# Attention and two MLPs on one core: first loads in runs of tokens, products of the identity between TensorE's first jobs, another order of the first jobs and of the weights

## Chip, cores and metric

One core of a Trainium2 chip runs the whole program. The metric is device time in microseconds (us), the median of the runs of one kernel. The profile is of one execution. Its times count from the start of its span. The engines are PE (TensorE), DVE (VectorE), ACT (ScalarE), POOL (GpSimd) and SP (SyncE, which here only issues DMAs).

## What is computed

Inputs are float32: q, k and v are 2 x 8 heads x 768 tokens x 64. Three parts follow one another:

```
scores_l = q k^T / 8, kept where |i - j| < 16, else -1e9
scores_s = q max_over_blocks_of_32(k)^T / 8 + log 32
a = softmax(concat(scores_l, scores_s)); x = a concat(v, mean_over_blocks(v))
x -> (1536 x 512);  h = x @ w_in1;  x = (max(h,0) + alpha min(h,0)) @ w_out1
h = x @ w_in2;  g = (a0 + a1 h + a2 h^2 + a3 h^3) / (1 + |b0||h| + |b1|h^2);  out = g @ w_out2
```

w_in is 512 x 2048 and w_out 2048 x 512 in both MLPs.

## The kernel before, in words

Tokens are taken in four chunks of 384 (two halves of each of the two batches). An attention job is one pair of heads of one chunk: 16 jobs, of which 0 to 3 are chunk 0. A job has the stages KQ (L879: keys and queries are transposed on PE into PSUM, `transposes` at L871, and copied to `kt` and `qt` by ACT, L545; DVE takes the maxima over blocks, L736), KX (L896, the same for the keys that lie past the chunk's window, DVE at L743 and L731), SC (L903: scores, 12 products; DVE adds the mask and finds the maximum, L756; ACT takes the exponential, L571), NM (DVE divides by the sum, L760), TR (L913: the probabilities are transposed, ACT copies them to `pt`, L579), AV (L919: means of the values by one product with `avg`, copied by ACT in SU, L580), and PV (L926: 12 products with the values, ACT writes `x_hi` and DVE `x_lo`, L588 and L772).

The MLPs are computed in split precision: each weight is a high part (ACT, L597 and L603) and a low part (POOL, L505 and L510), and each product of 128 x 384 is three matmuls (L948 to L950). An MLP step i works on one tile f = i mod 16 of the hidden dimension: `hidden1(i)` is 12 matmuls, `output1(i - 2)` another 12. From step 0 on, the stages of the next chunk's jobs lie in slots between them. For chunk 1 `SOON` (L66) puts job 4's KQ in step 0, SC in step 2, TR and PV in step 3. In step f of chunk 0 ACT does the slots' work, then makes the high parts of some weights (`weights`, L664 to L668), and then copies `g1_hi` of the step (L673), all in this order. Before, step 2 makes the weights of tiles 5 and 6, step 3 those of 7 and 8, and step f from 4 on that of f + 5.

Chunk 0's four jobs have nothing to lie beside. Their stages run in three orders written out by hand, one list for each of PE, ACT and DVE (`FIRST_PE`, `FIRST_ACT`, `FIRST_DVE`, L69 to L78), with the products of `hidden1(0)` and `hidden1(1)` (HD) at PE's end, and the high parts of the weights 0 to 2 (WI, WO) in ACT's. Each of the four jobs has PSUM banks of its own. POOL makes the identity, which PE's transposes need, and the constants, then adds up the values of each pair (L472), then splits weights; `keep_first_sums` (L494) follows the first two.

SP issues every DMA in one order (L370 to L423). `load_pair` (L265) makes two DMAs, one for each head. In them each partition gets one token of each tile, so every packet is 64 floats (256 B). `load_w(0, n)` loads the weights of the tiles 2n and 2n + 1 (1 MB). `load_keys(5)` waits until PE has transposed the keys of job 4 (L286), and `load_values(4)` waits for `pool_v0` (L335), which `keep_first_sums` raises.

Of the kernel before, what the change touches and what calls it, by code (L numbers as in the profile page):

```python
# [13 lines left out]
def attention_two_mlps(nc, q, k, v, w_in1, w_out1, alpha, w_in2, w_out2, a_coef, b_coef, out):  # L14
# [10 lines left out]
    B, H, S, D = q.shape  # L25
    DM, DF = w_in1.shape
    P = 128
# [41 lines left out]
    FIRST_PE = [(0, KQ), (0, KX), (1, KQ), (0, SC), (1, KX), (2, KQ), (0, AV), (1, SC), (2, KX), (0, TR), (3, KQ),  # L69
                (2, SC), (1, TR), (1, AV), (0, PV), (3, KX), (2, AV), (3, SC), (2, TR), (3, AV), (1, PV), (2, PV),  # L70
                (3, TR), (0, HD), (3, PV), (0, HD), (0, HD), (0, HD), (1, HD), (1, HD), (1, HD), (1, HD)]

    FIRST_ACT = [(0, KQ), (1, KQ), (0, SC), (2, KQ), (0, SU), (1, SC), (0, TR), (3, KQ), (1, TR), (2, SC), (1, SU), (0, PV),
                 (2, SU), (0, WI), (2, TR), (3, SC), (1, PV), (3, SU), (3, TR), (2, PV), (1, WI), (3, PV),
                 (2, WI), (0, WO), (1, WO), (2, WO)]

    FIRST_DVE = [(0, KQ), (0, KX), (1, KQ), (0, SC), (1, KX), (0, NM), (2, KQ), (1, SC), (2, KX), (1, NM), (2, SC),
                 (3, KQ), (3, KX), (2, NM), (0, PV), (3, SC), (3, NM), (1, PV), (2, PV), (3, PV)]  # L78
# [25 lines left out]
    k_raw0 = place("k_raw0", [P, 4, H, D], offset=w_end - 4 * H * D * 4)  # L104
    kx_raw0 = place("kx_raw0", [P, 4, H, D], offset=w_end - 8 * H * D * 4)
    q_raw0 = place("q_raw0", [P, QTILES, H, D], offset=w_end - (8 + QTILES) * H * D * 4)
# [49 lines left out]
    with ExitStack() as ctx:  # L156
# [107 lines left out]
        def _(sp):  # L264
# [4 lines left out]

            def first_k(p):  # L270
                hs = heads(p)
                load_pair(k_raw0[:, :, hs, :], KROWS[0], k[0, hs, 0:4 * KROWS[0], :], k0_loaded[p])

            def first_q(p):
                hs = heads(p)
                load_pair(q_raw0[:, :, hs, :], P, q[0, hs, 0:CH, :], q0_loaded[p])

            def first_kx(p):
                hs = heads(p)
                load_pair(kx_raw0[:, :, hs, :], KXROWS, k[0, hs, 4 * KROWS[0]:S, :], kx0_loaded[p])  # L280
# [94 lines left out]
            first_rest(0)  # L375
            first_kx(1)
            first_k(2)
            first_q(2)
            first_rest(1)
            first_k(3)  # L380
            first_kx(2)
            first_q(3)
            first_rest(2)
            first_windows(0)
            first_edges()
            first_kx(3)
            first_rest(3)
            load_w_in(0, 0)
# [150 lines left out]
        def _(act):  # L539
# [109 lines left out]
            for i in range(STEPS):  # L649
# [14 lines left out]
                if c == 0:  # L664

                    for n in (f + 3,) if f < 2 else (2 * f + 1, 2 * f + 2) if f < 4 else (f + 5,):
                        if n < FT:
                            weights(0, n)  # L668
# [419 lines left out]
```

## Time and profile before

| | us |
|---|---|
| median of 3 runs | 626.73 |
| lowest and highest | 626.6, 627.32 |
| the profiled execution | 627.17 |
| its span | 625.5 |
| TensorE busy | 608.0 |
| from the start to the end of step 0's products | 39.37 |
| the longest gap of TensorE after that, before 350 us | 3.22 |

A page of the profile has busy times, a line of 40 slices, and the chain of work that ended last. The windows give the same for any stretch, with the clock that was granted to TensorE, as a share of its full 2.4 GHz (0.50 is 1.2 GHz). In the timeline a row is one instruction or several alike: start, duration, engine, line, operation, tile written and tiles read, count, and in brackets how long the engine had been idle and what released it. A product of float32 tiles (L910, L925, L938) shows as two MATMUL rows, a transpose (L875, L917) as one.

### The profile page before, as it was taken

The numbers are of one execution on the slowest core, as the hardware profiler recorded it, in microseconds if no ns is written. First come the engines' busy times: TensorE is split into PE (matmuls) and PEld (weight loads), VectorE is DVE, ScalarE is ACT, GpSimd is POOL, SyncE is SP. The second block draws the span as 40 slices with busy tenths as digits, with TensorE's granted clock in tenths as the row PEclk, the third lists the DMA queues.
The fourth block names the chain that finished last, engine by engine and source line by source line (L and its number), as shares of the span: only waits on it lengthen the run. The fifth ranks groups of instructions, "written<-read, shape, count | busy, mean of one in ns | idle before, by whom it ended". The sixth has DMA issues, their size and how long they took to land.

```text
span 625.5 us, 10573 instructions
## 1 busy us (share of the span) xinstructions
PE 608.0 (97%) x3897; PEld 566.8 (91%) x3897; DVE 415.2 (66%) x953; ACT 312.7 (50%) x778; POOL 196.9 (31%) x221
## 2 busy tenths in 40 slices
PE   6897999999999999999999999999999999999997
PEld 4787999999999999999999989998998999899996
DVE  3663555556655554555555599877987788778775
ACT  4785453243223432332443487557656666656654
POOL 5467548000000000000322376443344334434431
PEclk9898999999999999999999999999999999999999
DMA  8979717202220222001444300001000000001001
GB/s 180 235 193 286 176 27 136 46 18 63 62 50 7 46 50 51 2 1 35 135 135 135 102 1 1 1 0 52 0 2 1 34 18 1 0 2 50 1 2 50
DMA packets 79539, 37.30 MB, mean 60 GB/s; under 512 B 56496, under 2 KB 72896, under 8 KB 79296
## 3 DMA queue, kind: packets, MB, share of 16 engines
q1 hardware_dynamic: 79488, 36.63, 23.1%
q8 instruction: 31, 0.51, 0.3%
q14 instruction: 20, 0.16, 0.1%
HBM read 32.58 MB, written 3.15 MB: 57 GB/s over the span
## 4 chain that ended last, share of the span: by engine, by line
PE 92%; SPq 3%; DMA 1%; DVE 1%; ACT 1%; issue 1%; ACTq 0%
PE acc L948 15%; PE acc L950 14%; PE acc L949 14%; PE hid L948 11%; PE hid L950 10%; PE hid L949 10%; PE att L948 4%; PE att L950 4%; PE att L949 4%; SPq L268 2%; PE att L938 2%; PE att L875 1%; PE att L910 1%; PE att L917 1%; DMA w_out_raw<-in_moe_w_out_dram 1%; DMA kx_raw<-in_k_dram 1%
## 5 line engine op out<-in xcount | busy, mean ns | idle before, releaser
L948 PE MATMUL hid<-x_hi,w_in_hi 128*128 128x384 f32 x384 | 130.7, 340 | 0.0
L950 PE MATMUL hid<-x_hi,w_in_lo 128*128 128x384 f32 x384 | 129.3, 337 | 0.0
L949 PE MATMUL hid<-x_lo,w_in_hi 128*128 128x384 f32 x384 | 129.3, 337 | 0.0
L510 POOL TENSOR_TENSOR w_out_lo<-w_out_raw,w_out_hi 128x512 fp32r<-128x512 f32 x32 | 41.3, 1292 | 226.1 <-ACT w_out_hi L541 225.9
L948 PE MATMUL acc<-g_hi,w_out_hi 128*128 128x384 f32 x256 | 91.0, 356 | 0.0
L531 POOL TENSOR_SCALAR qpart<-habs,ab 128x384 f32<-128x384 f32 x64 | 44.0, 688 | 143.1 <-ACT poly L690 142.4
L950 PE MATMUL acc<-g_hi,w_out_lo 128*128 128x384 f32 x256 | 86.8, 339 | 0.0
L949 PE MATMUL acc<-g_lo,w_out_hi 128*128 128x384 f32 x256 | 86.5, 338 | 0.0
L541 ACT ACTIVATE g_hi<-hid 128x384 fp32r<-128x384 f32 x96 | 48.3, 503 | 69.3 <-PE acc L950 62.0
L788 DVE TENSOR_TENSOR g_lo<-hid,g_hi 128x384 fp32r<-128x384 f32 x64 | 35.6, 556 | 69.3 <-ACT g_hi L541 69.3
L950 PE MATMUL acc<-w_out_hi,g_lo 128*128 128x512 f32 x192 | 76.1, 396 | 0.0
L949 PE MATMUL acc<-w_out_lo,g_hi 128*128 128x512 f32 x192 | 75.6, 394 | 0.0
L948 PE MATMUL acc<-w_out_hi,g_hi 128*128 128x512 f32 x192 | 75.5, 393 | 0.0
L948 PEld LDWEIGHTS hid<-x_hi,w_in_hi 128*128 128x128 f32 x384 | 72.3, 188 | 1.9 <-DVE x_lo L772 0.4
L949 PEld LDWEIGHTS hid<-x_lo,w_in_hi 128*128 128x128 f32 x384 | 72.4, 189 | 1.3
L950 PEld LDWEIGHTS hid<-x_hi,w_in_lo 128*128 128x128 f32 x384 | 72.3, 188 | 0.0
L811 DVE TENSOR_SCALAR g_neg<-hid,prelu_alpha 128x384 f32<-128x384 f32 x64 | 39.4, 615 | 46.0 <-PE hid L950 46.0
L533 POOL TENSOR_TENSOR qpart<-qpart,habs 128x384 f32<-128x384 f32 x64 | 65.7, 1026 | 5.3
L948 PEld LDWEIGHTS acc<-g_hi,w_out_hi 128*128 128x128 f32 x256 | 48.0, 188 | 2.7 <-issue 1.7
L949 PEld LDWEIGHTS acc<-g_lo,w_out_hi 128*128 128x128 f32 x256 | 48.2, 188 | 0.0
L950 PEld LDWEIGHTS acc<-g_hi,w_out_lo 128*128 128x128 f32 x256 | 48.1, 188 | 0.0
L571 ACT ACTIVATE att<-att,nmax 128x120 f32<-128x120 f32 x78 | 24.7, 367 | 45.8 <-DVE nmax L756 45.8
(155 smaller groups left out, 1150.5 us busy)
## 6 DMA issues: line engine op xcount, KB each, us to landing
w_in_raw<-in_moe_w_in_dram SPq DMA_DIRECT2D x32, 256.0 KB, 4.3
w_out_raw<-in_moe_w_out_dram SPq DMA_DIRECT2D x16, 512.0 KB, 4.5
vw<-in_v_dram SPq DMA_DIRECT2D x32, 120.0 KB, 3.9
q_raw<-in_q_dram SPq DMA_DIRECT2D x32, 96.0 KB, 2.6
out_dram<-out_sb SPq DMA_DIRECT2D x12, 256.0 KB, 2.0
k_raw<-in_k_dram SPq DMA_DIRECT2D x16, 104.0 KB
k_raw<-in_k_dram SPq DMA_DIRECT2D x16, 100.0 KB
vs_raw<-in_v_dram SPq DMA_DIRECT2D x2, 768.0 KB, 7.9
```

Of the source, the lines that this page charges most:

```text
L268: sp.dma_start(dst[0:rows, :, h, :], src[h].rearrange("(t p) d -> p t d", p=rows)).then_inc(loaded, 16)
L510: pool.tensor_tensor(w_out_lo[:, f, :], w_out_raw[:, f, :], w_out_hi[f][:, :].bitcast(F32), ALU.subtract).then_inc(pool_w_out, 1)
L531: pool.tensor_scalar(qpart[:, i % 2, :], habs[:, i % 2, :], ab[:, 5:6], ab[:, 4:5], ALU.mult, ALU.add).then_inc(pool_qb, 1)
L533: pool.tensor_tensor(qpart[:, i % 2, :], qpart[:, i % 2, :], habs[:, i % 2, :], ALU.mult).then_inc(pool_q, 1)
L541: return act.activation(dst, src, ACT.Identity)
L571: last = act.activation(scores_of(bk, h, n), scores_of(bk, h, n), ACT.Exp, scale=-1.0, bias=nmax[:, s, i:i + 1], accum_out=sums_of(bk, h)[ ...
L788: dve.tensor_tensor(g1_lo[:, i % R1, :], hid[i % 2][:, 0:CH], g1_hi[:, i % R1, :].bitcast(F32), ALU.subtract).then_inc(dve_g, 1)
L811: dve.tensor_scalar(g_neg[:, :], hb, 0.0, prelu_alpha[:, f:f + 1], ALU.min, ALU.mult).then_inc(dve_m, 1)
L938: last = pe.matmul(bk[0][rows, u * QT:(u + 1) * QT], values, pt[0:KU, s, h * UP + u // 2, tokens], start=True, stop=True)
L948: pe.matmul(dst, lhs[0], rhs[0], start=start, stop=False)
L949: pe.matmul(dst, lhs[0], rhs[1], start=False, stop=False)
L950: return pe.matmul(dst, lhs[1], rhs[0], start=False, stop=stop)
```

## The change

The first loads of keys and queries become one DMA for each pair, in which a partition gets a run of 4 (queries: 3) neighbouring tokens of each head. What a transpose writes then goes to every fourth (third) column. The two heads are transposed one by one, by a product with the identity whose result has 64 partitions. Products of the identity with itself, 15 in all, are issued ahead of four of PE's first jobs, into a bank that is not yet used. The three lists and SP's order are new, and in chunk 0 ACT makes the weights of tile f + 3 in step f, one tile in each step.

```diff
     SOON = {(0, 2): [KQ], (2, 0): [SC], (2, 2): [NM], (3, 0): [TR], (3, 2): [PV]}
-    FIRST_PE = [(0, KQ), (0, KX), (1, KQ), (0, SC), (1, KX), (2, KQ), (0, AV), (1, SC), (2, KX), (0, TR), (3, KQ),
-                (2, SC), (1, TR), (1, AV), (0, PV), (3, KX), (2, AV), (3, SC), (2, TR), (3, AV), (1, PV), (2, PV),
-                (3, TR), (0, HD), (3, PV), (0, HD), (0, HD), (0, HD), (1, HD), (1, HD), (1, HD), (1, HD)]
-    FIRST_ACT = [(0, KQ), (1, KQ), (0, SC), (2, KQ), (0, SU), (1, SC), (0, TR), (3, KQ), (1, TR), (2, SC), (1, SU), (0, PV),
-                 (2, SU), (0, WI), (2, TR), (3, SC), (1, PV), (3, SU), (3, TR), (2, PV), (1, WI), (3, PV),
+    FIRST_PE = [(0, KQ), (0, KX), (1, KQ), (0, SC), (1, KX), (1, SC), (2, KQ), (0, AV), (0, TR), (2, KX), (3, KQ),
+                (1, AV), (2, SC), (1, TR), (3, KX), (2, AV), (0, PV), (3, SC), (2, TR), (1, PV), (3, AV), (3, TR),
+                (2, PV), (3, PV), (0, HD), (0, HD), (0, HD), (0, HD), (1, HD), (1, HD), (1, HD), (1, HD)]
+    RUN_UP = {(0, KQ): 5, (0, KX): 3, (1, SC): 4, (0, AV): 3}
+    FIRST_ACT = [(0, KQ), (1, KQ), (0, SC), (2, KQ), (1, SC), (0, SU), (0, TR), (3, KQ), (1, SU), (1, TR), (2, SC),
+                 (2, SU), (0, PV), (2, TR), (3, SC), (0, WI), (3, SU), (3, TR), (1, PV), (2, PV), (1, WI), (3, PV),
                  (2, WI), (0, WO), (1, WO), (2, WO)]
-    FIRST_DVE = [(0, KQ), (0, KX), (1, KQ), (0, SC), (1, KX), (0, NM), (2, KQ), (1, SC), (2, KX), (1, NM), (2, SC),
-                 (3, KQ), (3, KX), (2, NM), (0, PV), (3, SC), (3, NM), (1, PV), (2, PV), (3, PV)]
+    FIRST_DVE = [(0, KQ), (0, KX), (1, KQ), (1, KX), (0, SC), (1, SC), (0, NM), (2, KQ), (1, NM), (2, KX), (3, KQ),
+                 (2, SC), (3, KX), (2, NM), (3, SC), (0, PV), (3, NM), (1, PV), (2, PV), (3, PV)]
     top = (nc.sbuf_base + 31) // 32 * 32
...
     w_in_raw = place("w_in_raw", [P, FT, KD, P], offset=top)
     w_in_lo = place("w_in_lo", [P, FT, KD, P], F32R)
     w_end = top + FT * DM * 4
-    k_raw0 = place("k_raw0", [P, 4, H, D], offset=w_end - 4 * H * D * 4)
-    kx_raw0 = place("kx_raw0", [P, 4, H, D], offset=w_end - 8 * H * D * 4)
-    q_raw0 = place("q_raw0", [P, QTILES, H, D], offset=w_end - (8 + QTILES) * H * D * 4)
+    k_raw0 = place("k_raw0", [P, H, 4, D], offset=w_end - 4 * H * D * 4)
+    kx_raw0 = place("kx_raw0", [P, H, 4, D], offset=w_end - 8 * H * D * 4)
+    q_raw0 = place("q_raw0", [P, H, QTILES, D], offset=w_end - (8 + QTILES) * H * D * 4)
     w_out_hi = [place(f"w_out_hi{f}", [P, DM], F32R) for f in range(FT)]
     w_out_raw = place("w_out_raw", [P, FT, DM], offset=top)
     w_out_lo = place("w_out_lo", [P, FT, DM], F32R)
...
                 for h in range(2):
                     sp.dma_start(dst[0:rows, :, h, :], src[h].rearrange("(t p) d -> p t d", p=rows)).then_inc(loaded, 16)
+            def load_runs(dst, rows, src, loaded):
+                sp.dma_start(dst[0:rows, :, :, :].rearrange("p h t d -> p h (t d)"),
+                             src.rearrange("h (p t) d -> p h (t d)", p=rows)).then_inc(loaded, 16)
             def first_k(p):
                 hs = heads(p)
-                load_pair(k_raw0[:, :, hs, :], KROWS[0], k[0, hs, 0:4 * KROWS[0], :], k0_loaded[p])
+                load_runs(k_raw0[:, hs, :, :], KROWS[0], k[0, hs, 0:4 * KROWS[0], :], k0_loaded[p])
             def first_q(p):
                 hs = heads(p)
-                load_pair(q_raw0[:, :, hs, :], P, q[0, hs, 0:CH, :], q0_loaded[p])
+                load_runs(q_raw0[:, hs, :, :], P, q[0, hs, 0:CH, :], q0_loaded[p])
             def first_kx(p):
                 hs = heads(p)
-                load_pair(kx_raw0[:, :, hs, :], KXROWS, k[0, hs, 4 * KROWS[0]:S, :], kx0_loaded[p])
+                load_runs(kx_raw0[:, hs, :, :], KXROWS, k[0, hs, 4 * KROWS[0]:S, :], kx0_loaded[p])
             def load_keys(j):
                 b, hs, n = batch(j), heads(pair(j)), KROWS[half(j)]
...
             first_kx(0)
             first_k(1)
             first_q(1)
-            first_rest(0)
             first_kx(1)
             first_k(2)
+            first_rest(0)
+            first_kx(2)
             first_q(2)
             first_rest(1)
             first_k(3)
-            first_kx(2)
             first_q(3)
             first_rest(2)
+            first_kx(3)
             first_windows(0)
             first_edges()
-            first_kx(3)
             first_rest(3)
-            load_w_in(0, 0)
             first_windows(1)
             sp.dma_start(alpha_rows[0:FT, :], alpha.rearrange("(f p) -> f p", p=P)).then_inc(alpha_loaded, 16)
+            load_w_in(0, 0)
             first_windows(2)
             first_windows(3)
             load_w_out(0, 0)
...
             load_keys(4)
             load_w_out(0, 1)
             load_w(0, 2)
+            load_w(0, 3)
+            load_values(4)
+            load_w(0, 4)
             load_keys(5)
-            load_values(4)
-            load_w(0, 3)
-            load_w(0, 4)
             load_w(0, 5)
             load_values(5)
             load_w(0, 6)
...
                 slot(c + 1, f, 2)
                 if c == 0:
-                    for n in (f + 3,) if f < 2 else (2 * f + 1, 2 * f + 2) if f < 4 else (f + 5,):
-                        if n < FT:
-                            weights(0, n)
+                    if f + 3 < FT:
+                        weights(0, f + 3)
                 if i >= LAST + LW:
                     weights(1, i - LAST - LW)
                 if i >= R1:
...
                 def transposes(dst, raw, raw0, rows, tiles):
+                    columns = dst[:, 0:rows * tiles].rearrange("p (r t) -> p r t", t=tiles)
                     for t in range(tiles):
-                        rows_of_pair = raw0[0:rows, t, heads(p), :] if first else raw[0:rows, t, :, :]
-                        tr = pe.transpose(dst[:, t * rows:(t + 1) * rows], rows_of_pair.rearrange("p h d -> p (h d)"), ident[0:rows, 0:rows])
+                        if first:
+                            for h in range(2):
+                                tr = pe.matmul(columns[h * D:(h + 1) * D, :, t], raw0[0:rows, 2 * p + h, t, :], ident[0:rows, 0:rows],
+                                               start=True, stop=True)
+                        else:
+                            tr = pe.transpose(dst[:, t * rows:(t + 1) * rows], raw[0:rows, t, :, :].rearrange("p h d -> p (h d)"),
+                                              ident[0:rows, 0:rows])
                     return tr
                 before = j - 1 if j > NPAIR else 0
...
                     if j == 0:
                         pe.wait_ge(pool_ready, 1)
                     if first:
-                        pe.wait_ge(k0_loaded[p], 32)
+                        pe.wait_ge(k0_loaded[p], 16)
                     else:
                         pe.wait_ge(dve_x, before + 1)
                         pe.wait_ge(k_loaded, 32 * (j - NPAIR + 1))
                     transposes(bk[0], k_raw, k_raw0, n, 4).then_inc(pe_k, 1)
                     if first:
-                        pe.wait_ge(q0_loaded[p], 32)
+                        pe.wait_ge(q0_loaded[p], 16)
                         if j == 3:
                             pe.wait_ge(act_su, 1)
                     else:
...
                 elif stage == KX and half(j) == 0:
                     pe.wait_ge(dve_kmax, kx_jobs(j))
                     if first:
-                        pe.wait_ge(kx0_loaded[p], 32)
+                        pe.wait_ge(kx0_loaded[p], 16)
                     else:
                         pe.wait_ge(kx_loaded, 32 * (kx_jobs(j) - NPAIR))
                     transposes(bk[0], kx_raw, kx_raw0, KXROWS, 4).then_inc(pe_kx, 1)
...
                         mm.then_inc(pe_y, 1)
             begun = [0, 0]
+            pe.wait_ge(pool_ready, 1)
             for j, stage in FIRST_PE:
+                for _ in range(RUN_UP.get((j, stage), 0)):
+                    pe.matmul(acc[2][:, 0:P], ident[:, :], ident[:, :], start=True, stop=True)
                 if stage == HD:
                     hidden1(j, [begun[j]])
                     begun[j] += 1
```

## Rows read from the trace of the kernel before

**Rows 1.** The page: busy tenths and granted clock in 40 slices.
```profile
PE   6897999999999999999999999999999999999997
...
PEclk9898999999999999999999999999999999999999
```
**Rows 2.** Windows: stretch, length, busy us of each engine, PEclk, DMA share, GB/s.
```profile
0.00:17.00 17.00, 9.96 (x80) 7.62 (x81) 7.57 (x36) 7.64 (x25) 9.65 (x26) 1.00 0.82 183
...
39.37:50.72 11.35, 11.35 (x87) 10.27 (x86) 6.49 (x24) 7.30 (x24) 8.80 (x8) 1.00 0.67 173
50.72:53.94 3.22, 0.00 (x1) 0.04 (x1) 0.88 (x2) 1.77 (x4) 2.12 (x2) 0.98 1.05 344
53.94:57.40 3.46, 3.46 (x30) 3.34 (x31) 1.33 (x3) 1.88 (x4) 0.79 (x1) 0.52 1.13 330
57.40:67.40 10.00, 10.00 (x80) 9.55 (x80) 5.31 (x20) 4.81 (x16) 6.75 (x6) 1.00 0.99 230
```
**Rows 3.** The chain that ended last: start, us, what.
```profile
46.91 5.09 DMA w_out_raw<-in_moe_w_out_dram
...
73.54 0.85 PE att L938 x24
```
**Rows 4.** Timeline, ACT and PE around 52 us.
```profile
52.02 0.63 ACT L541 ACTIVATE w_out_hi<-w_out_raw 128x512 fp32r<-128x512 f32 x1 [1.75 <-DMA w_out_raw<-in_moe_w_out_dram]
...
52.93 0.86 ACT L541 ACTIVATE pt<-att 120x384 f32<-120x384 f32 x2
...
53.94 1.55 PE L938 MATMUL att<-pt,vw 120*64 120x64 f32 x24 [3.22 <-ACT pt L541]
```
**Rows 5.** Waits of SP's own queue, 0 to 80 us: total, times, longest.
```profile
SPq L268 <- PE att L875: 9.5, 2, 5.1
```
**Rows 6.** Timeline, DVE: first reduction of KX, then all its waits to 36.3 us.
```profile
7.29 0.53 DVE L743 TENSOR_REDUCE att<-att 128x11 f32<-128x352 f32 x1 [0.94 <-PE att L875]
...
9.04 0.60 DVE L736 TENSOR_REDUCE hid<-hid 128x13 f32<-128x416 f32 x1 [0.78 <-ACT kt L541]
...
11.40 0.29 DVE L756 CUSTOM_DVE_ANT_0 att<-att,mask 128x120 f32<-128x120 f32 x1 [1.76 <-PE att L910]
...
17.69 0.53 DVE L743 TENSOR_REDUCE acc<-acc 128x11 f32<-128x352 f32 x1 [0.28 <-PE acc L875]
...
21.74 0.29 DVE L756 CUSTOM_DVE_ANT_0 acc<-acc,mask 128x120 f32<-128x120 f32 x1 [1.40 <-PE acc L910]
...
24.75 0.53 DVE L743 TENSOR_REDUCE acc<-acc 128x11 f32<-128x352 f32 x1 [1.00 <-PE acc L875]
...
28.69 0.29 DVE L756 CUSTOM_DVE_ANT_0 acc<-acc,mask 128x120 f32<-128x120 f32 x1 [0.82 <-PE acc L910]
...
31.55 0.16 DVE L764 TENSOR_SCALAR pden<-acc 128x3 f32<-128x3 f32 x1 [1.31 <-ACT acc L571]
...
35.01 0.56 DVE L772 TENSOR_TENSOR x_lo<-acc,x_hi 128x384 fp32r<-128x384 f32 x1 [1.11 <-ACT x_hi L541]
...
36.21 0.56 DVE L772 TENSOR_TENSOR x_lo<-acc,x_hi 128x384 fp32r<-128x384 f32 x1 [0.65 <-ACT x_hi L541]
```
**Rows 7.** Timeline, start: SP's first loads, identity, TensorE's jobs; scores late.
```profile
0.82 0.87 SPq L268 DMA_DIRECT2D k_raw<-in_k_dram  x2
...
1.25 0.29 POOL L432 TENSOR_SCALAR_AFFINE_SELECT ident<-ident 128x128 f32<-128x128 f32 x1 [0.23 <-POOL ident L430]
...
4.05 0.93 PE L875 MATMUL att<-ident,k_raw 104*128 104x104 f32 x4 [4.05 <-DMA k_raw<-in_k_dram]
...
9.73 1.48 PE L910 MATMUL att<-kt,qt 64*64 64x120 f32 x24
...
21.61 1.53 PE L917 MATMUL hid<-ident,probs 128*120 128x128 f32 x6
...
22.93 0.48 PE L925 MATMUL att<-v_all_early,avg 96*120 96x128 f32 x2
...
64.50 0.85 PE L910 MATMUL att<-kt,qt 64*64 64x120 f32 x24
```
**Rows 8.** Windows of 0.25 us: where the granted clock fell and rose.
```profile
26.50:26.75 0.25, 0.25 (x1) 0.25 (x2) 0.22 (x3) 0.25 (x1) 0.17 (x2) 0.55 1.03 194
...
29.75:30.00 0.25, 0.25 (x3) 0.25 (x2) 0.25 (x4) 0.23 (x1) 0.25 (x1) 0.62 0.89 344
```
**Rows 9.** Windows of 2 us: the DMAs' GB/s (last column).
```profile
2.00:4.00 2.00, 0.00 (x0) 0.00 (x0) 0.00 (x0) 0.10 (x1) 1.71 (x6) 1.00 0.89 201
...
36.00:38.00 2.00, 2.00 (x13) 1.75 (x12) 0.91 (x3) 1.85 (x5) 1.78 (x3) 1.00 0.97 309
```

## The prediction, made before the changed kernel was run

> **What bounds the kernel now.** I read the page first: TensorE is at nine tenths in nearly every slice [rows 1], and from 57.4 us on it has work without a gap until the second MLP. A change that touches the start can only bring that point forward; what follows it keeps its length. So I read the windows up to there [rows 2]. In the first 17 us TensorE is busy for 9.96. Then two losses stand out: from 50.72 to 53.94 it does nothing for 3.22 us, and for the next 3.46 us it works at a granted clock of 0.52 (1.2 GHz for nearly all of it). The page shows the second as the dip in its fourth slice.
>
> The chain and the timeline tell what ended that gap. TensorE waited for ACT's copy of job 4's probabilities, ACT makes that copy only after the high part of weight tile 6, and that one waited for its load, 5.09 us on the chain [rows 3, 4]. The load stood in SP's queue behind the keys of job 5, for which SP waited up to 5.1 us on TensorE's transposes [rows 5]. So it is an order's fault, not bandwidth's.
>
> Before 39.37 us no one engine bounds. DVE comes nearest: from its first reduction of KX at 7.29 to the end of its last x_lo (36.21 + 0.56 = 36.77) it waits nine times, 9.11 us in all [rows 6], so 20.4 us are its own work. TensorE itself runs there at half speed: 12 products of the scores take 1.48 us at 9.73 and 0.85 at 64.50 [rows 7]. The column of the granted clock reads 1.00 at 9.73 all the same; its first recorded change is the fall at 26.5, with the rise at 29.9 [rows 8]. I go by the durations.
>
> **The change part by part.** Durations are of one execution of 627.17 us (span 625.5); the median is 0.44 below it, and I subtract the gain from the median.
>
> *The gap at 50.72.* Tile 6 is now made in step 3, behind TR and PV, and its load goes ahead of load_values(4) and load_keys(5). Both remove the wait. In step 2 ACT then has one tile (two copies) after job 4's exponentials, and the copies of job 4 are out before output1(1) ends at 50.7. TensorE goes straight from output1(1) into PV. That gives back 3.22 us. Since it doesn't stand still, its clock doesn't fall: 3.46 us at 0.52 would be 1.8 at full clock, 1.66 less [rows 2]; by the pieces (PV 1.55 against 0.85 [rows 3, 4], six later products) I get 1.5. I take 1.6, together **4.8**. Bounds: 3.2 if the clock falls anyway, 4.9 at most.
>
> What is late next: load_keys(5), now behind load_values(4) and 1 MB more of weights. At the 230 to 344 GB/s of these stretches [rows 2] that megabyte takes 3 to 4.5 us, and the keys are wanted only in step 4, about 14 us after step 0. SP's wait on TensorE is over by then, so this queue gets shorter. What stands behind a wait for pool_v0 in load_values(4) (load_w(0, 4), load_keys(5)) has the same 14 us. The later tiles are made three steps (some 15 us) ahead of use, and POOL's splitting of tile 4's outgoing weights stands behind tile 6's incoming ones for one step; output1(4) is two steps off. I cost these at nothing.
>
> *The first loads.* Twelve DMAs instead of 24, each issued in 0.43 (two in 0.87 [rows 7]), take 5.2 us off SP's queue, and 1 KB packets replace 256 B ones. The DMAs moved 201 GB/s while only the small packets ran and 309 with the weights' larger ones [rows 9]. I put the new packets near 309; lower bound 201. Keys of job 0 land at about 3.6, not 4.05. A job's three loads are 589 KB, 2.9 us at the one rate and 1.9 at the other, so the fourth job's land about 4 us earlier. At the lower bound the first jobs' end moves by only 0.2 us, because DVE and TensorE then set the pace.
>
> *The transposes of the first four jobs.* Seven for KQ become 14 products and four for KX eight. The trace has no such product. Nearest is PV: 12 products, K 120, 64 outputs, heads on alternate halves of the array, 768 columns in 0.85 us, or 1.55 at the half clock [rows 3, 4]: 1.1 or 2.0 ns a column. Keys (832 columns) then cost 0.92 or 1.6, queries (768) 0.85 or 1.5, KX (704) 0.78 or 1.4, where the old four transposes of keys took 0.93 at the half clock [rows 7]. So at full clock a new one costs what an old one costs at half; at half clock it is dear. Bounds: 0.85 ns, if long columns hide the overhead, and for the strided write in PSUM, which no row shows, up to double.
>
> *The 15 identity products.* The float32 product of AV, 128 columns, takes 0.48 [rows 7]; counted from start to start 0.43 cold, half of it warm. The first five run from 1.6 us, once the identity is there (1.25 + 0.29), to 3.8: 0.2 past the keys' landing. Of the other ten, three delay KX(0) by 0.25 and the rest fill waits. Their cost on the path is 0.4. What they are worth is the clock. It rose at 29.9 after 3.4 us without a gap in AV, SC and TR, and at 57.2 after PV and MLP products [rows 8, 2]; it did not rise between 9.7 and 13.4 us, where TensorE was as full, but mostly with transposes. Now it is full from 1.6 to 8 us, and with products alone. I take the rise at about 6 us; bounds 4 and 12.
>
> The Trainium skill ("TensorE: Matmul & The Clock Gate", PE-mode transpose) says that transposes don't count as activity for this clock. This trace agrees with it for the stretch of 9.7 to 13.4; without the rule a rise as late as 12 us would be as good a guess as 6, and step 0 would end 2.6 later.
>
> *The first jobs worked forward.* Each job gets its duration from these rows and starts at the latest of its engine's previous job and what it waits for, plus 0.07. With the old lists and landings this ends step 0 at 38.75, where the trace has 39.37, so I add 0.6. With the new lists: KQ(0) 3.8 to 6.5, KX(0) 7.2 to 8.0, KQ(1) to 9.8, SC(0) to 10.5, KX(1) to 11.3, SC(1) 12.6 to 13.4, SC(2) ending at 21.4, SC(3) at 25.0. DVE begins KX(0)'s reduction at 8.25, 0.96 later than before. After it come the same 20.4 us of work and waits of 0.74 (keys 1), 1.15 (KX 1), 0.09, 0.67 (SC 2), 0.15, 1.73 (PV 1, behind TR 3) and 0.4, in all 4.9 where there were 9.1. It ends at 8.25 + 20.4 + 4.9 = 33.6, against 36.77. Step 0 ends at 36.4, with the 0.6 at 37.0: **2.4 us earlier**. Of this most is order and landings: with the new lists and loads but the old transposes and clock I get the same 36.5. A warm clock and dearer products nearly cancel.
>
> *Sum:* 2.4 + 4.8 = 7.2 on 627.17; less 0.1 for a hop or two in the slots is 7.1. From the median, 626.73 - 7.1 = **619.6**.
>
> **Rivals.**
>
> *The clock falls once more or rises late* (0.22). Between 24 and 30 us TensorE still has only some 2.5 us of work, with a gap of 1.7. Before, the clock fell at 26.5 after a stretch like it [rows 8]. A fall at 30 makes PV and HD slow and costs 1.3 by the same working; a first rise at 12 instead of 6 costs 2.6. Gain 4.5 to 5.8: 621 to 622.3. Against it: nothing in the list guards that place, so it is quite possible.
>
> *Another wait takes the gap's place* (0.1). ACT in step 3 or PV for its values, whose DMAs now run beside 2 MB of weights: 344 GB/s and a DMA share over 1 in the gap say that the DMAs are full there [rows 2]. A third to a half of the 4.8 would stay: 621.5 to 622.5. If the whole gap stayed and only the first jobs gained, 624.3.
>
> *The new transposes are dearer than PV's products* (0.12), the one on the other side. Each writes every fourth or third column of PSUM. At 1.5 times the price the forward working ends step 0 at 39.4 + 0.6, at double at 43.6 + 0.6, at triple at 52.8 + 0.6. Double makes the change worth 4.8 - 4.8 = 0 (626.7); triple gives 636. It decides from about 1.9 times. Against it: the two heads write different halves, as in PV, and at 1.1 ns a column they write PSUM less often than the MLPs' products do (most of 80 matmuls with 384 columns each in 10 us [rows 2]).
>
> The Trainium skill ("PSUM — Partial Sum Buffer", Specifications) says that any non-contiguous access pattern slows matmuls significantly. No row before shows such a pattern written by TensorE; by that sentence the sum would be this rival's, and its 0.12 is my doubt of it here.
>
> *The change does less than it says* (0.04): the loads in runs land no earlier and the lists wait elsewhere. Only the 4.8 remains: 622.
>
> **How the numbers follow.** The forecast has 0.52; its own bounds (rise at 4 or 8 us, 0.85 ns a column, the middle's 4.5 to 4.9) give 618.3 to 620.8. The range goes down to 617.8 and up to 624.3, over the first two rivals and the milder half of the third. Left out are the whole doubled price and a gain beyond every bound, under 0.2. A measurement can tell 0.2%, 1.25 us, from no change. Slower by more than that needs over twice the price per column: 0.06. Within it: 0.04. Faster: 0.90.
>
> **What would show it.** Right: no wait of TensorE's PV for ACT in step 3, and no DMA wait of ACT at L541 there; a granted clock of 1.00 from 45 to 60; scores of job 0 in about 0.8 us, not 1.48; end of step 0's products at 37 (36 to 39). KX's eight products in 0.7 to 0.9 us warm prove the price; 1.4 or more warm would be the PSUM rival. DVE's waits up to the last x_lo should sum to about 5. A second window of 0.50 near 30 would be the first rival. The forecast is wrong if step 0 ends after 39.4 or any gap over 1 us stands between it and 57 us; from 60 us on both traces should be alike, only shifted.

## The result and the profile after

The changed kernel takes 620.94 us (620.12 to 621.24 in 4 runs), the kernel before 626.79. The ratio is 0.9896, with a 95% interval of 0.9874 to 0.9918. That is 5.85 us less, where 7.1 were forecast (619.6). The profiled execution took 620.91, its span 619.2.

The page of the changed kernel, busy tenths and granted clock:

```profile
PE   8899999999999999999999999999999999999997
...
PEclk9989999999999999999999999999999999999999
```

Before, the clock dips in the second and in the fourth slice [rows 1]. Both dips are gone; one is there in the third slice, at 31 us. Two instructions mark off the stretches in both traces: the first transposes of job 4 (the end of step 0's products) and of job 5 (step 4). First the timeline of PE before, then after:

```profile
39.54 0.51 PE L875 MATMUL att<-ident,k_raw 100*128 100x100 f32 x4
...
58.45 0.51 PE L875 MATMUL att<-ident,k_raw 100*128 100x100 f32 x4
```

```profile
38.06 0.51 PE L886 MATMUL att<-ident,k_raw 100*128 100x100 f32 x4
...
52.22 0.51 PE L886 MATMUL att<-ident,k_raw 100*128 100x100 f32 x4
```

Call the first instant X, the second Y. X comes 1.48 us earlier, the stretch from X to Y shrinks from 18.91 to 14.16, 4.75 less, and from Y to the end of the span it is 567.05 against 566.98. So nothing happened after Y, and 1.48 + 4.75 = 6.23 is the spans' difference to 0.07. The forecast had 2.4 and 4.8.

Windows of the changed kernel (stretch, length, busy us of PE, PEld, DVE, ACT and POOL, PEclk, DMA share, GB/s) answer to those of [rows 2] and to the first 2 us window of [rows 9]:

```profile
0.00:17.00 17.00, 15.11 (x199) 13.10 (x199) 7.07 (x38) 7.01 (x27) 9.31 (x25) 1.00 0.85 209
2.00:4.00 2.00, 2.00 (x10) 1.80 (x9) 0.00 (x0) 0.10 (x1) 1.71 (x6) 1.00 0.75 230
8.00:10.00 2.00, 2.00 (x45) 1.96 (x44) 0.93 (x3) 0.38 (x2) 0.00 (x0) 1.00 1.09 254
31.25:34.50 3.25, 3.25 (x36) 3.00 (x31) 1.66 (x4) 2.61 (x6) 1.76 (x2) 0.50 0.94 222
38.06:52.22 14.16, 14.16 (x122) 13.08 (x121) 8.80 (x29) 9.62 (x29) 8.58 (x7) 1.00 0.98 258
```

From X to Y TensorE is busy without a gap at full clock: the stand at 50.72 and the slow 3.46 us behind it are both gone. From 31.25 on it runs at 1.2 GHz for some 3.3 us. The DMAs in the first stretch move 230 and 254 GB/s, not the 309 that I put them near.

The timeline of DVE after, with its first reduction of KX and the waits until its last x_lo, answers to [rows 6]:

```profile
8.90 0.53 DVE L749 TENSOR_REDUCE att<-att 128x11 f32<-128x352 f32 x1 [1.71 <-PE att L883]
...
10.35 0.60 DVE L742 TENSOR_REDUCE hid<-hid 128x13 f32<-128x416 f32 x1 [0.48 <-ACT kt L548]
...
11.88 0.53 DVE L749 TENSOR_REDUCE hid<-hid 128x11 f32<-128x352 f32 x1 [0.93 <-PE hid L883]
...
20.77 0.60 DVE L742 TENSOR_REDUCE acc<-acc 128x13 f32<-128x416 f32 x1 [0.32 <-ACT kt L548]
...
21.53 0.29 DVE L762 CUSTOM_DVE_ANT_0 acc<-acc,mask 128x120 f32<-128x120 f32 x1 [0.17 <-PE acc L922]
...
28.07 0.16 DVE L770 TENSOR_SCALAR pden<-acc 128x3 f32<-128x3 f32 x1 [0.48 <-ACT acc L578]
...
31.66 0.56 DVE L778 TENSOR_TENSOR x_lo<-hid,x_hi 128x384 fp32r<-128x384 f32 x1 [1.72 <-ACT x_hi L548]
...
33.68 0.56 DVE L778 TENSOR_TENSOR x_lo<-acc,x_hi 128x384 fp32r<-128x384 f32 x1 [1.00 <-ACT x_hi L548]
...
36.25 0.62 DVE L817 TENSOR_SCALAR g_neg<-hid,prelu_alpha 128x384 f32<-128x384 f32 x1 [1.93 <-PE hid L962]
```

The waits up to 34.24 sum to 0.48 + 0.93 + 0.32 + 0.17 + 0.48 + 1.72 + 1.00 = 5.1 (forecast 4.9, before 9.1). They begin from 8.90 (forecast 8.25) and the last x_lo ends at 34.24 (33.6). The last row shows what the slow clock does: DVE stands another 1.93 us for the first hidden tile, whose matmuls run at half speed.

TensorE's early jobs on the timeline after, to set beside [rows 7]:

```profile
4.17 1.66 PE L883 MATMUL att<-ident,k_raw 104*64 104x104 f32 x16
...
8.03 0.83 PE L883 MATMUL att<-ident,kx_raw 88*64 88x88 f32 x16
8.69 0.89 PE L883 MATMUL hid<-ident,k_raw 104*64 104x104 f32 x16
...
10.16 0.84 PE L922 MATMUL att<-kt,qt 64*64 64x120 f32 x24
```

Job 0's scores take 0.84 us instead of 1.48, so the clock is at full speed there; KQ of job 0 still ran slow. A KX of 704 columns takes 0.66 from start to start (8.03 to 8.69), which is 0.94 ns a column.

### The profile page after: what moved, and what is told of

Same layout as the page of the kernel before. It is cut to its first block, busy times and chain, and to the rows that moved or that the text cites. A ratio compares the mean times of both kernels' runs of the same rounds, so it can differ in the third digit from the quotient of the medians.

```text
span 619.2 us, 10885 instructions
## 1 busy us (share of the span) xinstructions
PE 610.2 (99%) x4059; PEld 569.6 (92%) x4059; DVE 414.0 (67%) x953; ACT 311.4 (50%) x778; POOL 197.3 (32%) x221
## 4 chain that ended last, share of the span: by engine, by line
PE 96%; DVE 3%; ACT 0%; issue 0%; POOL 0%; POOLq 0%
PE acc L960 15%; PE acc L962 14%; PE acc L961 14%; PE hid L960 11%; PE hid L962 11%; PE hid L961 11%; PE att L960 4%; PE att L962 4%; PE att L961 4%; PE att L950 2%; PE att L922 2%; PE att L886 2%; PE att L929 1%; PE att L883 1%; PE acc L1047 1%; DVE probs L774 1%
```

## The experiments

Twelve kernels were run, in three groups of four, each group with its own runs of the kernel before: medians of 627.03, 626.81 and 627.10 us there. The kernel before is not very steady on those chips (624.3 to 629.4 in 36 runs); differences under 1 us between kernels of different groups are not read. The first group ran on one chip, the second and the third on another. Each kernel's profile gives X, Y and the span:

| | median | X | Y | Y - X | span - Y | granted clock under 1 before Y |
|---|---|---|---|---|---|---|
| before | 626.79 | 39.54 | 58.45 | 18.91 | 567.05 | 26.5 to 30, 54 to 57 |
| after | 620.94 | 38.06 | 52.22 | 14.16 | 566.98 | 31 to 35 |
| e1: before, weights' order and lead | 621.58 | 38.03 | 52.63 | 14.60 | 566.97 | none |
| e2: after, old order and lead | 626.63 | 37.59 | 58.20 | 20.61 | 566.90 | 30 to 34, 51 to 58 |
| e3: after, no identity products | 621.93 | 39.25 | 53.43 | 14.18 | 566.97 | 29.6 to 36.4 |
| e4: after, six more ahead of TR 3 | 620.78 | 36.42 | 51.27 | 14.85 | 567.03 | none |
| e5: e4, WO 2 in step 0 | 620.25 | 36.00 | 51.55 | 15.55 | 567.15 | none |
| e6: after, neighbouring columns | 621.13 | 36.57 | 51.12 | 14.55 | 567.28 | none |
| e7: after, old lists | 621.22 | 37.61 | 51.77 | 14.16 | 567.13 | 26 to 30 |
| e8: after, old first loads, transposes | 622.42 | 39.03 | 53.20 | 14.17 | 567.00 | 16 to 20, 30 to 37 |
| e9: before, SP's order alone | 621.43 | 38.00 | 53.70 | 15.70 | 567.00 | none |
| e10: before, ACT's lead alone | 621.82 | 37.85 | 53.01 | 15.16 | 566.99 | none |
| e11: e5, keys 5 ahead of weights | 619.26 | 35.74 | 50.42 | 14.68 | 566.98 | none |
| e12: after, again | 620.85 | 38.29 | 52.45 | 14.16 | 566.95 | 31 to 35 |

The column span - Y is the same to 0.4 us in all of them: everything these edits do, they do before Y.

**e1, the weights alone.** The kernel before with

```diff
             load_w(0, 2)
-            load_keys(5)
-            load_values(4)
             load_w(0, 3)
+            load_values(4)
             load_w(0, 4)
+            load_keys(5)
...
-                    for n in (f + 3,) if f < 2 else (2 * f + 1, 2 * f + 2) if f < 4 else (f + 5,):
-                        if n < FT:
-                            weights(0, n)
+                    if f + 3 < FT:
+                        weights(0, f + 3)
```

> The kernel before with only SP's order of the weights and ACT's lead of three tiles changed; the first jobs are untouched. Theory A (the order of the weights is worth what the two traces show between the transposes of job 4 and those of job 5, 18.9 against 14.2 us): 626.8 - 4.7 = 622.1, no gap of PE near 51 us, step 0 ends at 39.4 as before. Rival (the wait comes back elsewhere once the first jobs end late, as loads are late too): over 624.

621.58 us (621.05 to 622.39, 4 runs), ratio 0.9925, interval 0.9902 to 0.9948: 5.45 us less than before. The gap is gone and Y - X is 14.60. X is 38.03 though the first jobs are the old ones, 1.5 earlier than in the profile of before, and no fall of the clock is recorded at 26.5. e9 and e10 (below), which keep the first jobs as well, have X at 38.00 and 37.85, again with no fall. In e10 nothing differs from the kernel before until step 2. In e9 DVE gets job 2's scores at 21.81, where the kernel before has 21.74 [rows 6]; behind the fall they part, and the wait of DVE that ends at 31.55 before ends at 30.03. So 1.5 us of X in the old kernel hang on whether the clock falls there in that execution. The two profiles that the first section compares differ in that as well as in the change.

**e2, the first jobs alone.** The changed kernel with e1's diff undone.

> The changed kernel with the old order of the weights behind load_w(0, 2) and the old lead of ACT. Theory A: only the first jobs' 1.5 us stay, 625.3, and a gap of about 3 us before job 4's PV is back, with the clock's fall behind it. Rival (the loads' lead from the faster start is enough to hide the wait): under 623.

626.63 us (625.24 to 628.95, 10 runs), ratio 1.0003, interval 0.9984 to 1.0021. Theory A held for the gap and missed the time. X is 1.95 us earlier than before, but Y is 58.20, only 0.25 earlier. The timeline of ACT shows why:

```profile
48.92 0.63 ACT L548 ACTIVATE w_in_hi<-w_in_raw 128x512 fp32r<-128x512 f32 x1 [2.78 <-DMA w_in_raw<-in_moe_w_in_dram]
...
51.20 0.63 ACT L548 ACTIVATE w_out_hi<-w_out_raw 128x512 fp32r<-128x512 f32 x1 [1.65 <-DMA w_out_raw<-in_moe_w_out_dram]
...
52.10 0.86 ACT L548 ACTIVATE pt<-att 120x384 f32<-120x384 f32 x2
```

ACT waits 2.78 and 1.65 us for the loads of tile 6, and job 4's copy comes at 52.10, where it came at 52.93 before. So PE stands for 4.34 us ahead of PV instead of 3.22, and the slow clock behind it lasts to 57.7. What ends the gap is a landing, not work. SP asks for job 5's keys 1.95 us earlier (38.13 against 40.08), but its DMAs of job 4's values then take longer to issue, and the load of tile 6's outgoing weights goes out at 46.20 against 46.91. A faster start mostly makes the wait longer. The half of the change that concerns the first jobs is worth nothing measurable without the other half.

**e9 and e10, the two parts of e1.** e9 has SP's order alone, e10 ACT's lead alone.

> The kernel before with SP's new order behind load_w(0, 2) alone; ACT keeps its old lead. Theory A (either half removes most of the gap: the load of tile 6 lands some 6 us earlier, so ACT doesn't wait for it in step 2): 622 to 623. Rival (ACT's two tiles in step 2 are themselves too much work ahead of g1_high(2) and job 4's copies): 624 to 625.5, with a shorter gap at 50 us.

> The kernel before with ACT's lead of three tiles alone; SP keeps its old order. Theory A (tile 6 is asked for in step 3, behind TR, and its load has landed by 52): the gap of PV is gone, but g1_high(3) waits for the load; 622.5 to 624.5. Rival (the wait only moves behind PV and costs the same): 625 to 627.

621.43 us (620.5 to 622.39) and 621.82 (621.67 to 625.32), ratios 0.9902 (0.9879 to 0.9925) and 0.9926 (0.9900 to 0.9953). Both are better than either theory had it, and neither can be told from e1. One of the two is enough. In e10 the load is still late, but it is asked for after the copies. The timeline of ACT in e10:

```profile
47.61 0.87 ACT L541 ACTIVATE pt<-att 120x384 f32<-120x384 f32 x2
...
52.70 0.63 ACT L541 ACTIVATE w_out_hi<-w_out_raw 128x512 fp32r<-128x512 f32 x1 [0.78 <-DMA w_out_raw<-in_moe_w_out_dram]
```

The copies of job 4 come at 47.61, and the wait for tile 6's load has shrunk to 0.78, at a place where PE has hidden1(4) to do. Both profiles have a stand of PE ahead of hidden1(2), behind a late load_w_out(0, 1) for which ACT waits (1.78 us in e9, 1.91 in e10). PE in e9, then in e10:

```profile
40.43 0.41 PE L948 MATMUL hid<-x_hi,w_in_hi 128*128 128x384 f32 x1 [1.59 <-DVE g_lo L788]
```

```profile
39.70 0.41 PE L947 MATMUL hid<-x_hi,w_in_hi 128*128 128x384 f32 x1 [1.01 <-DVE g_lo L787]
```

Without this stand Y - X would be 14.11 in e9 and 14.15 in e10; e1, whose stand is 0.46, has 14.14. That is the 14.16 of the changed kernel, where PE doesn't stand. So each of the two parts takes away the whole gap, and what their profiles have above 14.2 is the landing of load_w_out(0, 1), a limit that e4 meets again.

**e3, no identity products.** The changed kernel with

```diff
-    RUN_UP = {(0, KQ): 5, (0, KX): 3, (1, SC): 4, (0, AV): 3}
+    RUN_UP = {}
```

> The changed kernel without the 15 products of the identity. Theory A (the products bring the clock up at 7 us; without them the new transposes, being products, bring it up some us later): 0.5 to 2 us slower than the changed kernel, 621.5 to 623. Rival B (without them the clock stays at half until 20 us or more, and they are the whole gain of the start): 624 to 626. Rival C (they only fill waits): 620.9.

621.93 us (621.33 to 622.63, 4 runs), ratio 0.9930, interval 0.9907 to 0.9953: about 1 us above the changed kernel's two medians, inside theory A's range, though the intervals touch. The timeline of PE:

```profile
7.21 1.44 PE L883 MATMUL att<-ident,kx_raw 88*64 88x88 f32 x16
8.44 1.20 PE L883 MATMUL hid<-ident,k_raw 104*64 104x104 f32 x16
9.47 0.82 PE L883 MATMUL hid<-ident,q_raw 128*64 128x128 f32 x12
...
28.86 0.54 PE L929 MATMUL acc<-ident,probs 128*120 128x128 f32 x3 [1.21 <-DVE probs L774]
29.80 0.90 PE L929 MATMUL acc<-ident,probs 128*120 128x128 f32 x3 [0.39 <-DVE probs L774]
```

KX takes 1.44 us, then the keys of job 1 1.20 and its queries 0.82: the clock rises during these keys, about 9 us, where with the identity products KX at 8.03 was already fast. That is one to two us later and costs almost nothing, since no identity products stand ahead of KX: scores of job 0 begin at 10.22 against 10.16. The keys of job 0 start at 4.13 here, released by their DMA, and at 4.17 in the changed kernel, just behind the five identity products. The real loss is later. TR of job 3 takes 0.54 for its first half and 0.90 for its second; the clock has fallen at 29.6, and it is back only at 36.4, where the changed kernel is slow from 31.2 to 34.6. X is 1.2 later. Why the fall is longer without the identity products, 20 us behind the last of them, no run shows.

**e4, TensorE kept busy ahead of the fall.** Five more identity products ahead of TR of job 3, one between its halves, into `att[0]`, which is free there:

```diff
                     for g in range(2):
+                        if j == 3 and g == 1:
+                            pe.matmul(att[0][:, 0:P], ident[:, :], ident[:, :], start=True, stop=True)
                         pe.wait_ge(dve_p, 2 * j + g + 1)
...
+                if (j, stage) == (3, TR):
+                    pe.wait_ge(dve_x, 1)
+                    for _ in range(5):
+                        pe.matmul(att[0][:, 0:P], ident[:, :], ident[:, :], start=True, stop=True)
```

> The changed kernel with six more products of the identity: five before job 3's TR and one between its halves, where PE stands for 1.26 and 0.39 us ahead of the clock's fall at 31.2. Theory A (that stand brings the clock down, and the fall costs 1.3 to 1.7 us): the clock stays at full, 619.4. Rival (it falls anyway, since TR counts for little, or the products delay TR): 620.9 or a little above.

620.78 us (620.01 to 621.28, 4 runs), ratio 0.9910, interval 0.9887 to 0.9933. The clock never falls in the profile and X is 36.42, 1.64 us earlier than after: theory A's price of the fall at X, 1.3 to 1.7, is right. The products do hold the clock: e4, e5 and e11, which have them, ran 15 times, and 14 of these have a mean granted clock of 0.999 or 1.000; of the ten runs of the changed kernel without them (e12 among these) two have. But the stand does not bring the clock down each time, since e6 has the same stand, 1.27 and 0.39 us, and no fall in its profile. And the time hardly moves, where theory A had 619.4. Two rows of e4 tell where the gain went, ACT and then PE:

```profile
36.25 0.63 ACT L548 ACTIVATE w_out_hi<-w_out_raw 128x512 fp32r<-128x512 f32 x1 [1.73 <-DMA w_out_raw<-in_moe_w_out_dram]
...
38.00 0.41 PE L962 MATMUL hid<-x_hi,w_in_hi 128*128 128x384 f32 x1 [0.74 <-DVE g_lo L794]
```

ACT now waits 1.73 us for load_w_out(0, 1), the last weight in its first list, so g1 of step 0 is late and PE stands for 0.74 behind job 4's transposes. Y - X is 14.85 instead of 14.16. That takes back 0.7 in this execution; the other three ran 0.5 to 1.3 us longer than the profiled one.

**e5, that weight made later.** e4, and

```diff
-                 (2, WI), (0, WO), (1, WO), (2, WO)]
+                 (2, WI), (0, WO), (1, WO)]
...
+                    if f == 0:
+                        w_out_high(0, 2)
                     if f + 3 < FT:
```

> The kernel of e4 with the high part of outgoing weight tile 2 made in step 0, behind g1_high(0), instead of last in ACT's first list. Theory D (the landing of load_w_out(0, 1) at 36.2 now ends the first stretch: ACT waits 1.7 us for it, g1 of step 0 is late, and PE stands 0.74 us behind job 4's transposes): that stand is gone, 620.0. Rival (the stand moves to output1(0) or job 4's PV, which wait for other loads): 620.8.

620.25 us (619.47 to 621.85, 6 runs), ratio 0.9900, interval 0.9881 to 0.9919. The stand at 38 is gone, and two others are there. The rival was right that it would move, though it named other places. The last of them, on PE:

```profile
51.55 0.53 PE L888 MATMUL att<-ident,k_raw 100*128 100x100 f32 x4 [0.74 <-DMA k_raw<-in_k_dram]
```

PE stands 0.74 us for the keys of job 5, whose load the change put behind load_values(4) and 2 MB of weights, `load_w(0, 3)` and `load_w(0, 4)`. I had cost that order at nothing; with X two us earlier it isn't.

**e11, those keys ahead of the weights.** e5, and

```diff
             load_w(0, 3)
             load_values(4)
-            load_w(0, 4)
             load_keys(5)
+            load_w(0, 4)
```

> The kernel of e5 with load_keys(5) ahead of load_w(0, 4). Theory D (with the first jobs ended at 36, the landings set the next 15 us, and in e5 the last stand of PE, 0.74 us ahead of job 5's transposes, is for these keys): that stand is gone, the distance between the transposes of job 4 and of job 5 falls from 15.6 to 14.6 or less, 619.2. Rival (the DMAs are full and another load is late in its place): 620.2.

619.26 us (618.48 to 619.75, 5 runs), ratio 0.9872, interval 0.9854 to 0.9889. Y is 50.42, the earliest of all. Theory D's time was right; its "14.6 or less" for Y - X is 14.68. Of the stands behind X a wait of ACT for load_w_out(0, 2) and one of PE remain, ACT first:

```profile
39.98 0.63 ACT L548 ACTIVATE w_out_hi<-w_out_raw 128x512 fp32r<-128x512 f32 x1 [0.16 <-DMA w_out_raw<-in_moe_w_out_dram]
...
44.76 0.55 PE L933 MATMUL att<-ident,probs 128*120 128x128 f32 x3 [0.40 <-DVE probs L776]
```

**e12, the changed kernel beside it.**

> The changed kernel itself, unchanged, on the same chip as e9 to e11, so that one round of runs holds it beside them: 620.9, and if theory D holds 1 to 1.7 us above e11.

620.85 us (619.59 to 621.42, 6 runs), ratio 0.9895, interval 0.9878 to 0.9912. e11 is 1.6 us faster by the medians of one chip, the distance that theory D gave. Its slowest run is 0.16 above the fastest of e12, so the two distributions hardly overlap. e11 beats both kernels, by the six products, the later weight and the keys' order together.

**e6, the strided write.** The changed kernel with

```diff
-                    columns = dst[:, 0:rows * tiles].rearrange("p (r t) -> p r t", t=tiles)
+                    columns = dst[:, 0:rows * tiles].rearrange("p (t r) -> p r t", t=tiles)
```

> The changed kernel, in which the new transposes write neighbouring columns, so that the tokens of the first four jobs are in another order than they should be (the first chunk's attention is of other pairs of tokens). Theory A (the strided write costs nothing, the products' 0.85 to 0.94 ns a column is their own price): 88-column products of KX take 0.66 us from start to start as in the changed kernel, time 620.9. Rival (part of the price is the stride): 0.35 to 0.5 us for KX, and up to 1 us faster.

621.13 us (620.15 to 623.11, 4 runs), ratio 0.9914, interval 0.9890 to 0.9938, no gain. The timeline of PE:

```profile
7.98 0.83 PE L883 MATMUL att<-ident,kx_raw 88*64 88x88 f32 x16
8.64 0.89 PE L883 MATMUL hid<-ident,k_raw 104*64 104x104 f32 x16
9.36 0.83 PE L883 MATMUL hid<-ident,q_raw 128*64 128x128 f32 x12
```

KX takes 0.66 us from start to start, as with the stride, and the durations are the same, 0.83, 0.89 and 0.83. Writing every third or fourth column of PSUM costs these products nothing. X was 36.57 here, with no fall of the clock recorded, although PE stands ahead of job 3's TR as in the changed kernel.

**e7, the old lists.** The changed kernel with the three old lists.

> The changed kernel with the three old lists, the identity products kept ahead of the same four jobs. Theory A (the lists matter little once loads and clock are as they are): 620.5 to 621.5. Rival (the lists are what saves DVE's waits): 622 to 623.5.

621.22 us (620.46 to 623.17, 4 runs), ratio 0.9916, interval 0.9892 to 0.9941. Theory A: the new lists alone can't be told from the old. X is 37.61 with a fall of the clock in it, as the new lists have 38.06 with one.

**e8, the old first loads and transposes.** `load_pair` with its 256 B packets, and seven transposes for a KQ; lists, identity products and weights as changed.

> The changed kernel with the old first loads (24 DMAs, 256 B packets) and the old transposes; lists, weights and identity products are the new ones. Theory A (loads and transposes together are worth 1 us or more: later landings, a clock that rises late because transposes don't count): 622 to 623. Rival (the first jobs gain nothing by them): 620.5 to 621.3; then scores of job 0 take 0.85 us here too.

622.42 us (621.86 to 623.86, 5 runs), ratio 0.9940, interval 0.9919 to 0.9961; 1.2 and 1.3 above e7 and e6 on the same chip, as theory A had it, but not by a clock that rises late: job 0's scores take 0.85 us, the sign that was to speak for the rival. The timeline of PE:

```profile
6.30 0.53 PE L881 MATMUL att<-ident,kx_raw 88*128 88x88 f32 x4
...
8.14 0.85 PE L916 MATMUL att<-kt,qt 64*64 64x120 f32 x24
...
14.96 0.55 PE L881 MATMUL acc<-ident,q_raw 128*128 128x128 f32 x3 [2.88 <-DMA q_raw<-in_q_dram]
```

KX by transposes takes 0.53 at 6.30: the clock is up at least as early, with eight identity products around the transposes. Job 0's scores begin at 8.14, two us ahead of the changed kernel. Up to there the old way is better. Then the queries of job 2 land late, PE stands 2.88 us for them, the clock falls at 16.2, and X is 39.03. By this profile it is the loads in runs that pay, and the products in place of transposes are their price, since in `load_runs` the two heads of one token no longer lie side by side. e8 undoes both together, so this division is read from one trace and not measured.

## Why the prediction was right

*The gap at 50.72: 4.8.* Right, cause and size. Y - X fell by 4.75 in the profiles, e1 gives 5.45 by itself and e2 nothing. The forecast had both remove the wait and counted them once; e9 and e10 show that each alone does. Of the 4.8 the part of the clock, 1.6, is not in every execution: in four of the 36 runs of the kernel before the mean granted clock is 0.999 or 1.000, which leaves no room for a fall of 3.4 us (that would be 0.003 of the span), and these took 624.30 to 625.11, 2.0 to 2.5 us under the medians of their chips.

*What is late next.* I named load_keys(5) behind load_values(4) and 1 MB more of weights and cost it at nothing. The change puts it behind 2 MB, 6 to 9 us by the same rates, so the working was too short by half. In the changed kernel the nothing holds all the same (no stand before Y). e5 shows it as the next wait as soon as X is 2 us earlier, and e11 what it is worth. I did not name the one that came first, load_w_out(0, 1) at the end of ACT's first list (e4).

*The first jobs: 2.4.* This term was too large. By the profiles it is 1.48; by the medians it is 0.4 with the old weights (e2, 626.63 against 627.03) and about 0.7 with the new (e1's 621.58 against 620.94 and 620.85, on different chips). The order of the jobs in the three lists, to which the forecast gave most of this term together with the landings, is worth nothing measurable (e7). Three things took the rest. First, the start: I put the new packets near 309 GB/s and they ran at 230 to 254. Job 0's keys land at 4.13 (e3), where they landed at 4.05 before and I had 3.6, so they were transposed from 4.17 instead of 3.8. The clock rose later than the 6 us that I took: queries of job 0 take 1.45 from start to start and the three identity products behind them 1.00, where my price for a fast one, half of 0.43, makes 0.65. Together this puts KX at 8.03 instead of 7.2, and it is the 0.65 by which DVE began late. Second, the first rival came true beside the forecast: the clock fell once more, at 31.2, after 1.26 and 0.39 us of standing. PE in the changed kernel:

```profile
29.06 0.54 PE L929 MATMUL acc<-ident,probs 128*120 128x128 f32 x3 [1.26 <-DVE probs L774]
30.00 0.54 PE L929 MATMUL acc<-ident,probs 128*120 128x128 f32 x3 [0.39 <-DVE probs L774]
...
31.56 1.55 PE L950 MATMUL acc<-pt,vw 120*64 120x64 f32 x24
```

Its price was put at 1.3, and X is 1.64 earlier in e4 and 1.49 in e6. I had it as the less likely case, with 0.22; in both profiles of the changed kernel it is there, and by the mean granted clock eight of its ten runs have a fall somewhere. Third, the old kernel's own X, 39.54 in its profile, is 37.9 to 38.0 when the clock does not fall at 26.5 (e1, e9, e10). I took one execution's luck for the kernel's state.

*The forward working.* Its form was right, its hit in part luck. It ended step 0 at 36.4 with a clock that stays up, which is X at 36.6 (X was 0.17 later than that end before), and e4 and e6, where it stays up, have 36.42 and 36.57. But two errors cancel in it: in e4 DVE begins its first reduction of KX at 8.97 instead of 8.25, and waits 4.1 us in all instead of 4.9. The 0.6 that I added for the old lists' mismatch was not needed there.

*The identity products.* The rise came between 7.0 and 8.0 us (forecast 6), since the queries at 5.58 still ran slow, and the scores took 0.84. In the kernel before jobs run at half speed as late as 21.61 [rows 7]. But e3 has the rise at 9 without them and the same start of the scores, so they buy about 1 us (e3), and that by a fall of the clock 20 us later, which I did not foresee and of which no run shows the cause.

*The dearer products.* Their price a column was 0.94 and 0.85 ns (keys, 832 columns in the 0.71 from 8.69 to 9.40), under the 1.1 that I took and at the lower bound. The third rival, a price of 1.9 times by the stride, is excluded by e6.

*The rule on transposes.* The Trainium skill ("TensorE: Matmul & The Clock Gate", PE-mode transpose) says they don't count for the clock. The stretch of 9.7 to 13.4 before agreed. e3, where products take the transposes' place, has the clock up at 9, but its products are also longer and leave PE no gap, so it does not decide. e8 neither supports nor refutes it: after the identity products a mix of transposes, scores and more identity products kept the clock up until PE stood for 2.88 us. The rule on PSUM ("PSUM — Partial Sum Buffer", Specifications), that any non-contiguous pattern slows matmuls significantly, does not hold for these float32 products: 0.66 us with and without it.

So 7.1 forecast and 5.85 measured is a right middle and a start that gave a sixth to three fifths of what I took. The measured 620.94 lies 0.14 above what the forecast's own bounds give (618.3 to 620.8) and just under the first rival's 621, whose sign, a slow stretch near 30 us, is in the trace. What stays open is how much of the first jobs' half shows in the median of many runs: 0.4 to 1.5 us, since the fall of the clock comes and goes between executions in both kernels. An earlier start pays where the landings behind it are mended too: e11, which also has the six more products, is 7.84 us under the kernel before on its chip, e1 with the old first jobs 5.45 under it on its own.

## What to carry to other kernels

Ask of each gain at the start of a kernel what ends the next wait: if it is a landing in a full queue, an earlier start only lengthens that wait, and the order of the loads has to be mended first or with it (e2 against e1, e4 and e5 against e11). Where one engine both asks for loaded data and serves the bottleneck, either load earlier or ask later; one of them is enough. When clock falls of a few us come and go between executions, read from several profiles where they lie before a difference of one or two us is put down to a change.

## What had not been expected

- A write to every third or fourth column of PSUM costs float32 products nothing: 0.66 us for KX either way (e6).
- With packets of 1 KB the DMAs moved 233 to 246 GB/s from 2 to 9 us, in all nine kernels that have them; with 256 B it was 196 to 211, in the other five. Both are well under the 309 of the weights' loads. Whether the packets do it or the halved number of DMAs (SP takes 0.87 us to issue two, 0.43 for one) no run tells.
- The kernel before spreads over 5 us between executions on the two chips of the experiments (624.3 to 629.4), where the four of the first comparison agree to 0.7. The mean granted clock goes with the time: beside e9 to e12 its runs at 1.000 took 624.66 and 625.11, those at 0.989 took 628.08 to 628.90.
